# Attention, MoE and FFN on one core: the first numerators moved in front of the key-values, the last query transposes ahead of the last projection

## The reference

```python
def phi(x):                                   # x: (4, 8, 576, 64), w_phi: (64, 128)
    proj = np.einsum('bhsd,df->bhsf', x, w_phi)
    proj = proj - np.max(np.abs(proj), axis=-1, keepdims=True)
    return np.concatenate([np.exp(proj), np.exp(-proj)], axis=-1)
q_p, k_p = phi(q), phi(k)
kv  = np.einsum('bhsf,bhsd->bhfd', k_p, v)
z   = np.sum(k_p, axis=2)
num = np.einsum('bhsf,bhfd->bhsd', q_p, kv)
den = np.einsum('bhsf,bhf->bhs', q_p, z)[..., None] + 1e-06
x = num / den                                 # then (2304, 512)
# 2. a mixture of 8 experts (512 -> 1024 -> 512), the best expert of each token
# 3. a dense FFN (512 -> 2048 -> 512) with silu
```

## Time and profile before

| | |
|---|---|
| median of 3 runs | 906.73 us (904.99 to 908.0) |
| the profiled execution, its own time | 905.62 us |
| its span from first to last instruction | 903.7 us |
| mean granted TensorE clock | 0.993 |
| attention's steady rounds, one group | 11.12 us |

### The profile page before, as it was taken

How to read it: one execution, slowest core, us unless ns; L and a number is a source line. 1 busy time by engine, 2 the same in 40 slices (tenths; PEclk the granted TensorE clock), 3 DMA queues, 4 the chain that set the end, 5 groups by cost and what they waited for, 6 DMA issues and landing times.

```text
span 903.7 us, 18947 instructions
## 1 busy us (share of the span) xinstructions
PE 880.0 (97%) x6841; PEld 792.7 (88%) x6842; DVE 552.0 (61%) x822; ACT 431.2 (48%) x794; POOL 298.8 (33%) x265
## 2 busy tenths in 40 slices
PE   7999999978999998999999999999999999999997
PEld 6888888867888886888888889999999999999997
DVE  4767777758801599960090055562468898777882
ACT  4556655651444333433444465664666743333330
POOL 4686776633643455553453200000000011111111
PEclk9999999999999999999999999999999999999999
DMA  5455555416711578734111027645457545344421
GB/s 157 140 154 151 152 154 153 126 35 219 222 52 44 177 240 260 229 106 126 35 61 44 24 68 197 173 126 141 125 177 208 155 155 173 126 129 129 126 85 47
DMA packets 127445, 122.00 MB, mean 135 GB/s; under 512 B 35809, under 2 KB 102497, under 8 KB 127393
## 3 DMA queue, kind: packets, MB, share of 16 engines
q1 hardware_dynamic: 119680, 103.09, 39.3%
q0 software_dynamic: 3504, 11.28, 4.0%
q10 hardware_dynamic: 4208, 6.93, 2.1%
HBM read 86.39 MB, written 34.88 MB: 134 GB/s over the span
## 4 chain that ended last, share of the span: by engine, by line
PE 85%; SPq 4%; DVE 4%; issue 3%; DMA 2%; ACT 0%; POOL 0%; DVEq 0%; POOLq 0%; ACTq 0%
PE bank L712 22%; PE bank L714 22%; PE bank L713 22%; PE bank L786 4%; PE bank L726 3%; PE bank L740 3%; PE bank L913 2%; PE bank L707 2%; DVE w_hi L1526 2%; PE bank L767 2%; SPq L358 1%; PE bank L891 1%; PE bank L760 1%; PE bank L946 1%; SPq L360 1%
## 5 line engine op out<-in xcount | busy, mean ns | idle before, releaser
L695 POOL DMA_INDIRECT out<-temps,ids x18 | 25.1, 1395 | 325.4 <-DVE temps L1555 322.9
L666 POOL TENSOR_TENSOR h_lo<-h_raw,h_hi 128x512 fp32r<-128x512 f32 x49 | 73.1, 1513 | 157.7 <-ACT h_hi L1167 157.7
L712 PE MATMUL bank<-ops,place 128*128 128x384 f32 (+1 forms) x357 | 119.5, 335 | 1.3 <-DVE place L1654 1.1
L714 PE MATMUL bank<-ops,place 128*128 128x384 f32 (+1 forms) x357 | 118.3, 331 | 0.0
L713 PE MATMUL bank<-ops,place 128*128 128x384 f32 (+1 forms) x357 | 118.3, 331 | 0.0
L1617 DVE TENSOR_TENSOR temps<-temps,bank 128x384 f32<-128x384 f32 x72 | 39.8, 553 | 74.9 <-PE bank L714 74.5
L1526 DVE CAST w_hi<-ahead 128x1024 fp32r<-128x1024 f32 x48 | 48.5, 1011 | 56.8 <-PE bank L714 55.6
L712 PE MATMUL bank<-place,ops 128*128 128x256 f32 x294 | 83.2, 283 | 0.0
L713 PE MATMUL bank<-place,ops 128*128 128x256 f32 x294 | 83.2, 283 | 0.0
L714 PE MATMUL bank<-place,ops 128*128 128x256 f32 x294 | 83.2, 283 | 0.0
L712 PE MATMUL bank<-w_hi,xt_hi 128*128 x192 | 78.1, 407 | 2.7 <-DVE w_lo L1528 2.7
(11 more groups left out here) (239 smaller groups left out, 2196.8 us busy)
## 6 DMA issues: line engine op xcount, KB each, us to landing
ahead<-in_moe_w SPq DMA_DIRECT2D x56, 512.0 KB, 4.7
h_rows<-temps SPq DMA_DIRECT2D x96, 192.0 KB, 2.4
w_raw<-h_rows SPq DMA_DIRECT2D x17, 512.0 KB, 4.0
y_sorted<-y ACTq DMA_DIRECT2D x25, 256.5 KB, 2.9
raw<-h_rows SPq DMA_DIRECT2D x10, 512.0 KB, 3.7
tail<-h_rows SPq DMA_DIRECT2D x9, 512.0 KB, 3.7
qk<-in_k SPq DMA_DIRECT2D x32, 128.0 KB, 2.6
vs<-in_v SPq DMA_DIRECT2D x32, 128.0 KB, 2.3
```

The costliest lines, as they stand in the source:

```text
L666: nc.gpsimd.tensor_tensor(h_lo[:, fs, :], h_raw[:, fs, :], h_hi[:, fs, :].bitcast(F32), ALU.subtract).then_inc(h_lo_done, 1)
L712: mm(o, left_hi, right_hi, start=first, stop=False, skip_group_check=shared)
L714: return mm(o, left_lo, right_hi, start=False, stop=last, skip_group_check=shared)
```

## The change

On TensorE, in a round that has all three parts, `numerators(g - 1, 0)` moves from between the first two transposes to behind the projections of units 0 and 1, directly in front of `key_values(g)`. `transpose_queries(g, 2)` moves from behind `project(n, 2)` to in front of it. The features of query unit 0 of odd groups get a place of their own, `qT_other`, since the features of the next group are now written before the first numerators have read the old ones. ScalarE's order changes with it (`key_features(n, 1)` and then `move_pairs(n, 2)` ahead of `query_features(g, 1)`), and VectorE's (`shift(n, 0)` ahead of `normalize(g - 1, 0)`). A small integer tile of the routing is written to `ids` in place of `pos_hi`, which is gone. Nothing is computed otherwise than before, and no DMA is moved.

```diff
-        pos_hi = alloc(region, "pos_hi", [P, TS], I32)
+        qT_other = alloc(region, "qT_other", [P, PER_UNIT, 2, P])
...
+        def query_place(par, u):
+
+            return qT_other[:] if par and u == 0 else qT[:, PER_UNIT * u:PER_UNIT * (u + 1), :, :]
...
-                                      qT[:, s, c, 64 * m:64 * (m + 1)], kv[:, c, b if s else m, 0:DEN + 1],
+                                      query_place(par, s // PER_UNIT)[:, s % PER_UNIT, c, 64 * m:64 * (m + 1)], kv[:, c, b if s else m, 0:DEN + 1],
...
-                if prev:
-                    numerators(g - 1, 0)
+                if prev and not nxt:
+                    numerators(g - 1, 1 - par, 0)
...
                 if nxt:
                     project(n, npar, 0)
                     project(n, npar, 1)
+                if prev and nxt:
+                    numerators(g - 1, 1 - par, 0)
                 if cur:
                     key_values(g, par)
...
-                if nxt:
-                    project(n, npar, 2)
-                if cur:
                     if nxt:
                         pe.wait_ge(xT_moved, UNITS * n + 3)
                     else:
                         pe.wait_ge(exp_q_done, UNITS * g)
                     transpose_queries(g, par, 2)
+                if nxt:
+                    project(n, npar, 2)
...
                 if cur:
                     move_kvT(g)
+                if nxt:
+                    key_features(n, npar, 1)
                 if nxt and cur:
                     move_pairs(n, 2)
                 if cur:
-                    query_features(g, 1)
-                if nxt:
-                    key_features(n, npar, 1)
-                if cur:
-                    query_features(g, 2)
+                    query_features(g, par, 1)
+                    query_features(g, par, 2)
...
+                if nxt:
+                    shift(n, npar, 0)
                 if prev:
                     normalize(g - 1, 0, npar)
                 if nxt:
-                    shift(n, npar, 0)
                     shift(n, npar, 1)
...
-            step(tsc(pos_hi[:], pos[:], 7, None, ALU.logical_shift_right))
-            step(nc.vector.tensor_copy(hi_b[:], pos_hi[:]))
+            step(tsc(ids[:], pos[:], 7, None, ALU.logical_shift_right))
+            step(nc.vector.tensor_copy(hi_b[:], ids[:]))
```

More of the change, by code:

```diff
@@ L769, in transpose_queries, with numerators @@
                 last.then_inc(qT_done, 1)
-            def numerators(g, b, to=ps_num):
+            def numerators(g, par, b, to=ps_num):
                 if b == 0:
@@ L820, in attention @@
                 if prev:
-                    numerators(g - 1, 1)
+                    numerators(g - 1, 1 - par, 1)
                 if not nxt:
@@ L851, in _ @@
             attention(GROUPS - 1, 1, nxt=False)
-            numerators(GROUPS - 1, 0)
-            numerators(GROUPS - 1, 1, ps_last)
+            numerators(GROUPS - 1, 1, 0)
+            numerators(GROUPS - 1, 1, 1, ps_last)
             pe.wait_ge(hot_ready, 1)
@@ L1093, in key_features, with query_features @@
                 nc.scalar.activation(phi_k[npar][:, slots, 1, :], src, ACT.Exp, scale=-1.0).then_inc(exp_k_done, 1)
-            def query_features(g, u):
+            def query_features(g, par, u):
                 act.wait_ge(qT_done, UNITS * g + u + 1)
                 src = bank[:, ps_queries[u], 0:PER_UNIT * P].rearrange("p (s t) -> p s t", t=P)
-                slots = slice(PER_UNIT * u, PER_UNIT * (u + 1))
-                nc.scalar.activation(qT[:, slots, 0, :], src, ACT.Exp)
-                nc.scalar.activation(qT[:, slots, 1, :], src, ACT.Exp, scale=-1.0).then_inc(exp_q_done, 1)
+                to = query_place(par, u)
+                nc.scalar.activation(to[:, :, 0, :], src, ACT.Exp)
+                nc.scalar.activation(to[:, :, 1, :], src, ACT.Exp, scale=-1.0).then_inc(exp_q_done, 1)
             def attention(g, par, cur=True, nxt=True):
@@ L1107, in attention @@
                 if cur:
-                    query_features(g, 0)
+                    query_features(g, par, 0)
                 if nxt and not cur:
```

## The result

The changed kernel takes 908.82 us in the median of 19 runs beside 905.26 for the kernel before, also 19: 1.0035 of its time, 95% interval 1.0018 to 1.0051. By that ratio it is slower by 3.2 us, clear of no change; the two medians stand 3.6 us apart. The profiled execution has a span of 905.5 us, against 903.7.

A forecast was written before the change was run, and what follows sets the result against it. TensorE's gapless holds were taken to bound attention's rounds; 0.25 us lost in each of ten, plus both ends, made 2.9 us, giving 909.6 us against the 906.73 median, range 906.3 to 912.0.

The forecast's parts named there:

- The saving on TensorE: TensorE's holds in a steady round: fewer changes of array use cut their sum from 11.12 to 10.87 us, 0.25 less.
- N0: First numerators, `numerators(g - 1, 0)`, on TensorE; hold forecast to fall from 1.55 to 1.45 us in front of the key-values.
- What N0 covered: Ahead of Q0: ScalarE's copy of T0's unit, no longer hidden by N0, makes Q0 and what follows 0.47 to 0.54 us late.
- Q0: Query transposes of unit 0 on TensorE; due 0.71 us behind T0, forecast to start at 1.15 to 1.22, awaiting a copy.
- T0: Pair transposes of unit 0 on TensorE, from which a round is counted; hold forecast at 0.38 us instead of 0.42.
- The wait behind it: Ahead of P1: the wait for unit 2's shift, covered by 0.2 us with Q0's stop, a 0.25 us stop without it.
- P1: Projections of unit 1 on TensorE; due at 2.40 us behind T0 with Q0's stop, 1.90 without, released at 2.13 to 2.2.
- P0: Projections of unit 0 on TensorE, directly behind Q0; together with P1 forecast to keep their hold of 1.53 us.
- The move of Q2: End of a round on TensorE: Q2 ahead of unit 2's projections brings nothing by itself; last three steps stay 2.23 us.
- Q2: Query transposes of unit 2 on TensorE; due 10.0 us behind T0, their copy done at 9.5, so no stop forecast.
- T1: Pair transposes of unit 1 on TensorE; hold forecast 0.33 us instead of 0.38, with about 0.1 to spare awaiting Q2's features.
- How often it counts: Whole attention: ten rounds cost 2.5 us, round 14's rest 0.15, T0 of round 4 0.25 to 0.3 late; together 2.9.

The follow-up runs named there:

- e8: The e7 kernel with a group's values load also issued ahead of the stores of x; 0.9968 of the time before, mean round 10.85 us.
- e2: The changed kernel with the three transposes of T1 done twice in rounds 1 to 14; 906.87 us in one run, round 11.34 us.
- e4: The changed kernel with unit 0's query transposes written to the numerators' bank, so Q0 has no copy to wait for; 908.62 us in one run, round 11.28.
- e6: The changed kernel with key-values by feature cut in two, the second half and its VectorE copy behind T1 of the next round; 0.9992 of the time before.
- e9: The e8 kernel with round 14's key-values by feature left whole ahead of Q2; 900.71 us, 0.9952 of the time before.
- e10: The changed kernel with N0 back between T0 and T1 and VectorE's order of before; 0.9996 of the time before, round 11.17 us.
- e1: The changed kernel with Q2 back behind the last projection, ScalarE's order left; 912.29 us in one run, round 11.71 us.
- e5: The changed kernel itself, unaltered, timed and profiled again; 1.0026 of the time before, mean round 11.34 us.
- e7: The e6 kernel with the values' load waiting for the key sums instead of the key-values by feature; 0.9994 of the time before.

## Why the prediction held, by its steps

**The saving on TensorE: right.** Without its stop the round after is 10.88 (11.34 less 0.46), and e8 has 10.85 with the halves in it, against the sum's 10.87. N0 and the key-values hold 1.45 and 1.73 as forecast. The rows decide against the 0.1 a round that followed from the drain as the Trainium skill gives it (TensorEngine Tiling (Array Packing), Key Properties; TensorE: Matmul & The Clock Gate, step by step): the two changes fewer saved 0.24.

**What N0 covered: right, at the low end.** Q0 starts 1.12 behind T0, for 1.15 to 1.22 forecast, as the handover from the copy took 0.05 (104.53 to 104.58) and not up to 0.15. That longer one is seen in round 14, outside the loop, where Q0 is at 1.21. The second transpose behind the stop cost 0.05, not 0.03. Together Q0 and what follows is late by 0.46, for 0.47 to 0.54; the round is longer by 0.22 (0.21 on average of ten), the low end of 0.22 to 0.29. The trace names the copy, e2 shows that it isn't TensorE's own work, and e4 that Q0 is on time without it. "Nothing shorter can stand in for N0" was wrong: in e6 to e9 0.42 us of work do, where N0 has 1.55.

**The wait behind it: there, and under-priced.** P1's wait came out in e4 at its place. What the prediction missed is that P1, released from a stop, takes 0.13 more, and that P0 comes 0.06 late, so a free Q0 leaves not "next to nothing" of the 0.25 but a loss of 0.16.

**The move of Q2: the sentence that it brings nothing by itself was wrong,** though the sum was right, as it took the new T0 at 0.38. Alone it costs 0.05 a round (e10). With N0 moved it saves 0.37 (e1), since it clears ScalarE for the copy and T1. The prediction had that in its figures for ScalarE, but didn't draw the conclusion.

**How often it counts: right for the rounds, and by luck for the start.** Ten rounds cost 2.11 us, where 2.5 was forecast, and the rest of round 14 0.19 (0.15). The 0.32 at T0 of round 4 (0.25 to 0.3) agrees, but e5, the same kernel, is there 3.45 behind the kernel before. So no run shows that term, nor that the loads swallow three rounds' loss, though the chain does go over them. Attention's end moved by 2.6 (2.9) in one pair of profiles and by 5.7 in the other. One sign of being wrong, that attention's end and the span move by different amounts, did occur (2.6 and 1.8). It proved nothing, as what follows attention differs by up to 4.7 us between profiles. The measure that holds is the runs' ratio, 3.2 and 2.4 us in the two series for 2.9 forecast. The forecast time, 909.6, stood on a median before of 906.73 from three runs; with 19 it is 905.26, and 908.82 is 0.8 under the forecast.

## What to carry to other kernels

Before moving a step to save changes of the array's way of use, ask what it covered: here 1.55 us of numerators hid a copy of 0.48 and two handovers, and the move laid open twice what it saved (0.46 against 0.24). The cure was to put other work of the neighbours' kind, 0.42 us long, into the hole, and to issue the values' load earlier so that no round waits for loads. Compare the tail as well as the round, since a gap at the end of the loop can eat what the loop gained (e8 against e9). Before a difference at one point is put down to a change, see how far two profiles of the same kernel differ there: 3.1 us at round 4 here, and nothing in the length of a steady round.

## What the runs showed of the hardware

A stop costs more than its length. In the changed kernel the first two transposes behind one start 0.16 apart, and the next 0.11. In e4 a projection of twelve instructions behind one takes 0.90 instead of 0.77. A change of the array's way of use costs 0.10 at the change and 0.05 in the instructions behind it, and two changes fewer saved 0.24 a round. It isn't the same for all steps: e10 has as many changes as the kernel before, at other places, and its round is 0.05 longer.

In e8 TensorE had stopped for some 2 us, after P2 and a few matmuls, and then worked under a granted clock of 0.59 and 0.56 for 4 us, mostly the lower of its two levels, 1.2 GHz; the next 2 us had 1.00 (2.4 GHz) again. Forty instructions held 2.9 us there instead of 1.55. e6 and e7 have the same stop and a granted clock down to 0.50 behind it. The stops of 0.41 us in each round of the changed kernel left the clock at 1.00.
